# Scores of a chunk in one go on two row blocks of TensorE, the output gate loaded first, and the first values read one step earlier

## The chip, the cores and the metric

The kernel runs on one core of one Trainium2 chip. The metric is the device time of one execution in microseconds (us). Before the change it is 455.31 us as the median of three runs (453.54 to 456.17). The profiled execution took 455.49 us, of which the profile's span covers 453.8 us; the engines' names are PE (TensorE; PEld is its weight load), DVE (VectorE), ACT (ScalarE), POOL (GpSimd) and SP (SyncE, which only issues transfers here).

## The reference

An xLSTM-style attention with matrix memory, followed by a mixer (token mixing, then channel mixing). All numbers are float32; there are 4 batches, 8 heads, 768 tokens and a head size of 40, so the model width is 320.

```python
for t in range(S):                       # per batch and head
    m_new  = max(f_gate[t] + m, i_gate[t])
    f_stab = exp(f_gate[t] + m - m_new);  i_stab = exp(i_gate[t] - m_new);  m = m_new
    C = f_stab * C + i_stab * outer(v[t], k[t])          # 40 x 40
    n = f_stab * n + i_stab * k[t]
    y[t] = sigmoid(o_gate[t]) * (C @ q[t]) / max(|n . q[t]|, 1)
x  = y as (B, S, 320)
h  = relu(x^T @ w_tok1) @ w_tok2          # tokens: 768 -> 256 -> 768
u  = x + h^T
out = u + relu(u @ w_ch1) @ w_ch2         # channels: 320 -> 1536 -> 320
```

## The kernel before

**Chunks and steps.** The recurrence is computed in 6 chunks of 128 tokens (`NC`, `L`). Inside a chunk the tokens attend to each other: scores = keys times queries for each head, multiplied elementwise by decays `gb` (an exponential of gate sums), then multiplied by the values. Across chunks a state `st` per head is carried. A chunk is worked in three steps, one for each group of heads: 3, 3 and 2 heads (`HEADS`), so a batch has 18 steps (`STEPS`). Step m belongs to chunk m // 3 and group m % 3.

**Scores before.** `step_scores` makes one float32 matmul per step. The stationary operand is `kd`: the keys of the group's heads stacked on 120 (or 80) rows. The moving operand is `qz`: the queries laid out as blocks on the diagonal, each head's 40 rows beside zeros, 384 (or 256) columns wide. So one matmul gives the scores of three heads, and two thirds of its products are with zeros. In the trace a float32 matmul is two PE instructions, each with its own weight load. The result goes to PSUM bank `pS`; in batch 0 steps alternate between `pS` and `pC[0]`. `scores` on DVE reads the bank and multiplies it into `gb` (L856), one instruction per step. The zeros of `qz` are written once by DVE (L784), and SP waits for that (`mem_ready`) before it loads the first keys and queries, with one transfer for `kd` and three for `qz` per chunk.

**Other work of a step on PE.** `step_state` (L1089) makes the chunk's contribution to the state in bank `pN`, for step m - 1. `step_values` makes, for step m - 2, the product of queries and state (L1113) and of scores and values: in batch 0 one float32 matmul per head (L1124), in the later batches six bf16 ones per head (L1134), for which scores and values are split into three bf16 pieces by ACT (L628, L604), POOL (L494, L496) and DVE (`p_low`, L865).

**What runs beside what.** Every engine has a fixed list of instructions and works it in order; semaphores tie them. Batch 0's attention runs alone, up to about 51.6 us: there `spread_decays` (L1042, L1046) puts the decays into PSUM by matmul and ACT takes exponentials (L676), three steps ahead (`LEAD`). The attention of batch b + 1 is then spread over the mixer of batch b: for b = 0 all of it over the mixer's 24 slots, and for b = 1, 2 step 0 lies ahead of the second token matmul, step 1 inside it, and the others in slots 0 to 15. A slot is one tile of the hidden channel layer: `hidden` (8 matmuls, L1236 to L1241), then one attention step, then `project` of the slot before (9 matmuls, L1165); ACT and DVE split the hidden tile into two pieces between them (L760, L988). So 18 chunks of attention lie in mixers, and 6 stand alone.

**The start.** ACT issues the load of batch 0's output gate `o_gate` (two parts) and its first large instruction is the sigmoid of it (L580), ahead of all exponentials in ACT's list. DVE and POOL compute running sums of the gates on 32 rows in three segments (L794 maxima, L802 sums, L469 to L486 on POOL). PE runs idle matmuls (`keep_warm`, L1015) while it waits: 19, 5 and 10 of them at three places.

Of the kernel before, what the change touches and what calls it, by code (L numbers as in the profile page):

```python
# [50 lines left out]
FIRST_VALUES_AT = 6  # L51
# [8 lines left out]
WARM_START, WARM_NEXT, WARM_THIRD = 19, 5, 10  # L60
# [21 lines left out]
def program(nc, qT, kT, kvN, i_gate, f_gate, o_gate, w_tok1, w_tok2, w_ch1, w_ch2, out):  # L82
    ctx = ExitStack()
    with ctx:
# [25 lines left out]
        kd = sb("kd", [ROWS, R, NG, L])  # L110
        qz = sb("qz", [ROWS, R, NG, GH, L])
# [53 lines left out]
        def scores_bank(ba, m):  # L165

            return [pS, pC[0]][m % 2] if ba == 0 else pS
# [21 lines left out]
        mem_ready = sem("mem_ready")  # L189
# [114 lines left out]
        QK_DMAS = 4  # L304
# [4 lines left out]
        def _(sp):  # L309
# [3 lines left out]
            def load_scores(ba, c):  # L313

                n = NC * ba + c
                r = c % R
                if n >= R:
                    sp.wait_ge(s_mm, NG * (n - R + 1))
                ready = qk_in[r]
                queries = qT[ba, c]  # L320
                sp.dma_start(kd[:, r], kT[ba, c]).then_inc(ready, 16)
                for j in range(GH):
                    rows_j = slice(j * D, (j + 1) * D)
                    sp.dma_start(qz[rows_j, r, :, j, :], queries[rows_j, :, :]).then_inc(ready, 16)
# [60 lines left out]

            load_values(0, 0)
            sp.wait_ge(mem_ready, 1)
            load_scores(0, 0)
# [385 lines left out]
        def _(dve):  # L774
# [9 lines left out]
            nc.vector.memset(qz[:, :, :, :, :], 0.0).then_inc(mem_ready, 1)  # L784
# [63 lines left out]
            def scores(ba, m):  # L848

                c, g = divmod(m, NG)  # L850
                k = STEPS * ba + m
                n = HEADS[g]
                tile = gb[:, c % Q, GH * g:GH * g + n, :]
                dve.wait_ge(s_mm, k + 1)
                dve.wait_ge(e_exp, k + 1)
                nc.vector.tensor_tensor(tile, scores_bank(ba, m)[:, 0:n * L].rearrange("p (h t) -> p h t", h=n), tile,  # L856
                                        ALU.mult).then_inc(p_ready, 1)
# [10 lines left out]
            def state(ba, m):  # L868
# [6 lines left out]
                sums = pN[0:n * D, 0:n * E1].rearrange("p (h e) -> p h e", e=E1)  # L875
# [49 lines left out]
            def attention(ba, m):  # L925
# [3 lines left out]
                if 1 <= m <= STEPS - NG:  # L929
                    state(ba, m - 1)  # L930
# [77 lines left out]
        def _(pe):  # L1008
# [58 lines left out]
            def step_scores(ba, m):  # L1067

                c, g = divmod(m, NG)
                k = STEPS * ba + m  # L1070
                n, r = HEADS[g], c % R
                if g == 0:
                    pe.wait_ge(qk_in[r], 16 * QK_DMAS * (ba * (NC // R) + c // R + 1))
# [3 lines left out]
                mm(scores_bank(ba, m)[:, 0:n * L], kd[0:n * D, r, g, :],  # L1077
                   qz[0:n * D, r, g, 0:n, :].rearrange("p h t -> p (h t)"),
                   start=True, stop=True).then_inc(s_mm, 1)

            def step_state(ba, m):
# [5 lines left out]
                if ks != 0:  # L1087
                    pe.wait_ge(n_read, ks)
                mm(pN[0:n * D, 0:n * E1], kv[:, r, GH * g * D:(GH * g + n) * D],  # L1089
# [49 lines left out]
            def attention(ba, m):  # L1139

                if m < STEPS:
                    step_scores(ba, m)
# [10 lines left out]
                if 1 <= m <= STEPS - NG:  # L1153
                    step_state(ba, m - 1)
# [150 lines left out]
```

## Time and profile before

| what | value |
|---|---|
| time, median of 3 | 455.31 us (453.54 to 456.17) |
| profiled execution / its span | 455.49 us / 453.8 us |
| PE busy (weight loads) | 439.6 us, 97% (407.6 us, 90%) |
| DVE, ACT, POOL busy | 255.6, 209.1, 208.3 us |
| chain that ended last | PE 85%, DVE 5%, issue 4%, ACT 4% |
| score matmuls (L1077) | 144 PE instructions, two for each of the 72 steps |
| DVE's product with the scores (L856) | 72 instructions |

The page gives busy times as shares of the span, and the chain that ended last, traced back from the last instruction. A busy PE is not PE at its peak: a matmul's recorded duration holds its latency, and neighbours overlap. What one costs in a dense stretch is read from start to start. Two starts in a timeline give that.

### The profile page before, as it was taken

What the parts mean: (1) busy time and instruction counts of PE and PEld (TensorE: products, weight loads), DVE (VectorE), ACT (ScalarE), POOL (GpSimd) and SP (SyncE); (2) the same over time, 40 slices, a digit from 0 to 9 for tenths busy, and PEclk for the clock granted to TensorE, in tenths of its full rate; (3) what the DMA queues carried; (4) which work ended last, traced back from release to release, by engine and by line L of the source; (5) the groups of instructions that cost most, each with busy time, mean ns of one, the idle gap of its engine ahead of it and who ended that gap; (6) DMA issues with size and microseconds to landing.
All of it is one profiled execution on the core that took longest, in us unless ns stands there. A gap on an engine that the chain in (4) does not pass through costs nothing.

```text
span 453.8 us, 9518 instructions
## 1 busy us (share of the span) xinstructions
PE 439.6 (97%) x3463; PEld 407.6 (90%) x3463; DVE 255.6 (56%) x592; ACT 209.1 (46%) x517; POOL 208.3 (46%) x293
## 2 busy tenths in 40 slices
PE   8899999999999999899999999999999999999996
PEld 3588988999999989799999998899999998999996
DVE  7689865777765356776674237666665326213122
ACT  3666459666554247654552137655652213211120
POOL 7535421789886333888861204798883000000000
PEclk9899999999999999999999999999999999999999
DMA  7557990443344415434454013534310010000101
GB/s 211 195 168 217 348 263 27 119 129 111 103 131 146 127 43 166 143 92 131 124 154 143 1 44 102 150 120 142 126 61 1 1 43 2 0 1 0 46 1 43
DMA packets 36616, 47.38 MB, mean 104 GB/s; under 512 B 3356, under 2 KB 29082, under 8 KB 36570
## 3 DMA queue, kind: packets, MB, share of 16 engines
q1 hardware_dynamic: 35674, 45.76, 33.4%
q10 hardware_dynamic: 896, 1.02, 0.6%
q8 instruction: 28, 0.46, 0.5%
q14 instruction: 18, 0.15, 0.1%
HBM read 42.73 MB, written 4.03 MB: 103 GB/s over the span
## 4 chain that ended last, share of the span: by engine, by line
PE 85%; DVE 5%; issue 4%; ACT 4%; DMA 1%; DVEq 0%; POOL 0%; POOLq 0%; ACTq 0%
PE pC L1165 32%; PE pA L1236 7%; PE pA L1237 7%; PE pA L1238 7%; PE pS L1077 6%; PE pA L1165 5%; PE pY L1134 4%; PE pA L1240 3%; PE pA L1241 3%; PE pC L1015 2%; PE pY L1113 2%; PE pN L1089 2%; DVE gb L856 1%; PE pA L1195 1%; DMA x<-o_gate_dram 1%
## 5 line engine op out<-in xcount | busy, mean ns | idle before, releaser
L988 DVE SCALAR_TENSOR_TENSOR h_lo<-pA,h_hi 128x384 fp32r<-128x384 f32 x96 | 53.5, 557 | 147.9 <-ACT h_hi L760 147.9
L760 ACT ACTIVATE h_hi<-pA 128x384 fp32r<-128x384 f32 x96 | 46.8, 488 | 138.7 <-PE pA L1241 138.6
L1165 PE MATMUL pC<-wc_hi,h_hi 128*128 128x320 f32 x288 | 94.1, 327 | 1.1 <-DVE wc_lo L846 1.0
L1165 PE MATMUL pC<-wc_lo,h_hi 128*128 128x320 f32 x288 | 88.7, 308 | 0.0
L1165 PE MATMUL pC<-wc_hi,h_lo 128*128 128x320 f32 x288 | 88.4, 307 | 0.0
L494 POOL TENSOR_TENSOR gb<-gb,pb 128x384 f32<-128x384 f32 (+1 forms) x54 | 49.1, 909 | 63.9 <-ACT pb L628 63.4
L1236 PE MATMUL pA<-uT_hi,wc_hi 128*128 128x384 f32 x192 | 65.2, 340 | 0.3 <-DVE wc_lo L846 0.3
L1237 PE MATMUL pA<-uT_lo,wc_hi 128*128 128x384 f32 x192 | 64.7, 337 | 0.0
L1238 PE MATMUL pA<-uT_hi,wc_lo 128*128 128x384 f32 x192 | 64.3, 335 | 0.0
L1165 PEld LDWEIGHTS pC<-wc_hi,h_hi 128*128 128x128 f32 x288 | 54.0, 188 | 2.3 <-DVE h_lo L988 1.3
L1165 PEld LDWEIGHTS pC<-wc_lo,h_hi 128*128 128x128 f32 x288 | 54.2, 188 | 0.1
L1165 PEld LDWEIGHTS pC<-wc_hi,h_lo 128*128 128x128 f32 x288 | 54.0, 188 | 0.0
L618 ACT ACTIVATE gb<-gb,aT 128x128 f32<-128x128 f32 x144 | 47.4, 390 | 1.5 <-POOL gb L504 1.5
L1077 PE MATMUL pS<-qz,kd 120*128 120x384 f32 (+1 forms) x126 | 47.2, 455 | 0.5 <-DVE gb L856 0.5
L628 ACT ACTIVATE pb<-gb 128x384 bf16<-128x384 f32 (+1 forms) x54 | 26.3, 487 | 34.2 <-DVE gb L856 33.8
L865 DVE TENSOR_TENSOR pb<-gb,pb 128x384 bf16<-128x384 f32 (+1 forms) x54 | 38.1, 706 | 0.6
L526 POOL TENSOR_TENSOR x_lo<-x,x_hi 128x320 fp32r<-128x320 f32 x24 | 21.5, 897 | 33.3 <-ACT x_hi L652 33.3
L1236 PEld LDWEIGHTS pA<-uT_hi,wc_hi 128*128 128x128 f32 x192 | 36.2, 188 | 0.5 <-issue 0.5
L1238 PEld LDWEIGHTS pA<-uT_hi,wc_lo 128*128 128x128 f32 x192 | 36.1, 188 | 0.0
L1237 PEld LDWEIGHTS pA<-uT_lo,wc_hi 128*128 128x128 f32 x192 | 36.0, 188 | 0.0
L496 POOL CAST pb<-gb 128x384 bf16<-128x384 f32 (+1 forms) x54 | 31.4, 582 | 3.5
L856 DVE TENSOR_TENSOR gb<-pS,gb 128x384 f32<-128x384 f32 (+1 forms) x63 | 31.7, 503 | 1.2 <-PE pS L1077 0.8
(135 smaller groups left out, 881.6 us busy)
## 6 DMA issues: line engine op xcount, KB each, us to landing
gb<-g_dram SPq DMA_DIRECT2D x18, 512.0 KB, 3.9
kv<-kvN_dram SPq DMA_DIRECT2D x24, 324.0 KB, 4.0
kd<-kT_dram SPq DMA_DIRECT2D x24, 180.0 KB
qz<-qT_dram SPq DMA_DIRECT2D x72, 60.0 KB
out_dram<-u SPq DMA_DIRECT2D x24, 160.0 KB, 1.9
qd<-qT_dram SPq DMA_DIRECT2D x20, 180.0 KB, 2.6
gq<-g_dram SPq DMA_DIRECT2D x45, 60.0 KB
wc_raw<-w_ch_dram SPq DMA_DIRECT2D x6, 384.0 KB, 6.1
```

The costliest lines, as they stand in the source:

```text
L494: nc.gpsimd.tensor_tensor(tile, tile, pb[:, g, 0, 0:HEADS[g], :], ALU.subtract).then_inc(p_rest, 1)
L496: nc.gpsimd.tensor_copy(pb[:, g, 1, 0:HEADS[g], :], tile).then_inc(p_mid, 1)
L618: last = nc.scalar.activation(tile, tile, ACT.Exp, bias=aT[:, c, bass.ds(head, 1)])
L760: nc.scalar.activation(h2[0][:, slot % 2], pA[slot % 2][:, 0:HALF], ACT.Relu).then_inc(h2_hi, 1)
L856: nc.vector.tensor_tensor(tile, scores_bank(ba, m)[:, 0:n * L].rearrange("p (h t) -> p h t", h=n), tile, ALU.mult).then_inc(p_ready, 1)
L865: nc.vector.tensor_tensor(pb[:, g, 2, 0:n, :], gb[:, c % Q, GH * g:GH * g + n, :], pb[:, g, 1, 0:n, :], ALU.subtract).then_inc(p_split, 1)
L988: nc.vector.scalar_tensor_tensor(h2[1][:, slot % 2], pA[slot % 2][:, 0:HALF], 0.0, h2[0][:, slot % 2].bitcast(F32), ALU.max, ALU.subtract) ...
L1077: mm(scores_bank(ba, m)[:, 0:n * L], kd[0:n * D, r, g, :], qz[0:n * D, r, g, 0:n, :].rearrange("p h t -> p (h t)"), start=True, stop=True) ...
L1165: ins = mm(dst, a[p], b[q], start=first and n == 0, stop=last and n == 2)
L1236: mm(dst, wc1[0][:, t, f], uh[:, t, cols], start=t == 0, stop=False)
L1237: mm(dst, wc1[0][:, t, f], ul[:, t, cols], start=False, stop=False)
L1238: mm(dst, wc1[1][:, t, f], uh[:, t, cols], start=False, stop=False)
```

## The change

- Keys and queries are sent by the host in one array `kq_pairs`, with even heads on partitions 0 to 39 and odd heads on partitions 64 to 103 of a new tile `kq`; `kd`, `qz` and the memset of zeros are gone, and a chunk's load is 2 transfers of 40 partitions in place of 4.
- `chunk_scores` replaces `step_scores`: at the first step of a chunk it makes 8 float32 matmuls, one per head, each with 40 rows, 128 stationary and 128 moving columns, alternately on the upper and lower 64 rows. Even heads go to bank `pS`, odd heads to `pC[0]` in batch 0 and to `pN`, the state's bank, later. One semaphore count for all 8.
- It waits until DVE has read all scores of the chunk before; from batch 1 on also until DVE has read that chunk's states from `pN`.
- DVE reads each step's scores with two instructions, one for each bank.
- From batch 1 on the state matmuls move: none in a chunk's first step, group 0's in the second, groups 1 and 2 in the third (`states_in`, `state_place`), with waits both ways between scores and states in `pN`.
- SP waits for both parts of `o_gate` before it loads chunk 0's scores and values, in this order.
- `WARM_THIRD` goes from 10 to 8, and `FIRST_VALUES_AT`, the step at which DVE reads chunk 0's values, from 6 to 5.

```diff
-FIRST_VALUES_AT = 6
+FIRST_VALUES_AT = 5
-WARM_START, WARM_NEXT, WARM_THIRD = 19, 5, 10
+WARM_START, WARM_NEXT, WARM_THIRD = 19, 5, 8
...
-        kd = sb("kd", [ROWS, R, NG, L])
-        qz = sb("qz", [ROWS, R, NG, GH, L])
+        kq = sb("kq", [128, R, 2, H // 2, L])
...
+        def scores_place(ba, head):
+            pair, odd = divmod(head, 2)
+            return (pC[0] if ba == 0 else pN) if odd else pS, pair * L
+        def state_place(ba, g):
+            col = L if ba > 0 and g == NG - 1 else 0
+            return pN[0:HEADS[g] * D, col:col + HEADS[g] * E1]
+        def states_in(ba, m):
+            if ba == 0:
+                return [m - 1] if 1 <= m <= STEPS - NG else []
+            c, g = divmod(m, NG)
+            if c >= NC - 1 or g == 0:
+                return []
+            return [m - 1] if g == 1 else [m - 1, m]
...
-                    sp.wait_ge(s_mm, NG * (n - R + 1))
+                    sp.wait_ge(s_mm, n - R + 1)
-                sp.dma_start(kd[:, r], kT[ba, c]).then_inc(ready, 16)
-                for j in range(GH):
-                    sp.dma_start(qz[rows_j, r, :, j, :], queries[rows_j, :, :]).then_inc(ready, 16)
+                for odd in range(2):
+                    sp.dma_start(kq[64 * odd:64 * odd + D, r], kq_pairs[ba, c, odd]).then_inc(ready, 16)
...
+            sp.wait_ge(o_in[0], 16)
+            load_scores(0, 0)
+            sp.wait_ge(o_in[1], 16)
             load_values(0, 0)
-            sp.wait_ge(mem_ready, 1)
-            load_scores(0, 0)
...
-            nc.vector.memset(qz[:, :, :, :, :], 0.0).then_inc(mem_ready, 1)
...                                                   # DVE, scores(ba, m)
-                dve.wait_ge(s_mm, k + 1)
+                dve.wait_ge(s_mm, NC * ba + c + 1)
+                if ba > 0 and c < NC - 1 and g > 0:
+                    dve.wait_ge(n_mm, NG * (NC - 1) * ba + NG * c + (1 if g == 1 else NG))
                 dve.wait_ge(e_exp, k + 1)
-                nc.vector.tensor_tensor(tile, scores_bank(ba, m)[:, 0:n * L]..., tile, ALU.mult).then_inc(p_ready, 1)
+                for odd in range(2):
+                    heads = [h for h in range(GH * g, GH * g + n) if h % 2 == odd]
+                    ...
+                    last = nc.vector.tensor_tensor(tile, sums, tile, ALU.mult)
+                last.then_inc(p_ready, 1)
...                                                   # PE
-            def step_scores(ba, m):
-                held = 2 if ba == 0 else 1
-                if k >= held:
-                    pe.wait_ge(p_ready, k - held + 1)
-                mm(scores_bank(ba, m)[:, 0:n * L], kd[0:n * D, r, g, :],
-                   qz[0:n * D, r, g, 0:n, :]..., start=True, stop=True).then_inc(s_mm, 1)
+            def chunk_scores(ba, c):
+                n = NC * ba + c
+                if n > 0:
+                    pe.wait_ge(p_ready, NG * n)
+                if ba > 0:
+                    pe.wait_ge(n_read, states(ba, c - 1))
+                for head in range(H):
+                    pair, odd = divmod(head, 2)
+                    rows = slice(64 * odd, 64 * odd + D)
+                    last = mm(scores_of(ba, head), kq[rows, r, 0, pair, :], kq[rows, r, 1, pair, :],
+                              start=True, stop=True)
+                last.then_inc(s_mm, 1)
...                                                   # PE, step_state(ba, m)
+                if ba > 0:
+                    pe.wait_ge(p_ready, STEPS * ba + NG * c + (1 if g == 0 else 2))
+                    if g > 0:
+                        pe.wait_ge(n_read, NG * (NC - 1) * ba + NG * c + 1)
...                                                   # PE, attention(ba, m)
-                if m < STEPS:
-                    step_scores(ba, m)
+                if m < STEPS and m % NG == 0:
+                    chunk_scores(ba, m // NG)
```

PE's list in a mixer slot that holds the first step of a chunk (batch 1), before. `pS` and `pN` are the score and state banks, `pY` the values' bank.

```order
L1241 MATMUL pA<-uT_hi,wc_lo 128x384
L1077 MATMUL pS<-qz,kd 128x384
L1089 MATMUL pN<-vw,kv 80x82
L1113 MATMUL pY<-st,qd 128x123
L1134 MATMUL pY<-vb,pb 128x41 x18
```

The same place after the change.

```order
L1273 MATMUL pA<-uT_hi,wc_lo 128x384
L1104 MATMUL pS<-kq 128x128
L1104 MATMUL pN<-kq 128x128
L1104 MATMUL pS<-kq 128x128
L1104 MATMUL pN<-kq 128x128
L1104 MATMUL pS<-kq 128x128
L1104 MATMUL pN<-kq 128x128
L1104 MATMUL pS<-kq 128x128
L1104 MATMUL pN<-kq 128x128
L1145 MATMUL pY<-st,qd 128x123
L1166 MATMUL pY<-vb,pb 128x41 x18
```

One matmul of 384 columns became eight of 128, the two later steps of the chunk have none, and the state matmul left this slot for the chunk's third step.

DVE's list in batch 0 from the third step of chunk 2 to the first of chunk 3, before (`gb` holds the decays and takes the product, `stn` and `st` are the state).

```order
L856 TENSOR_TENSOR gb<-pS,gb 128x256
L886 TENSOR_TENSOR stn<-pN,blocks 120x123
L895 SCALAR_TENSOR_TENSOR st<-st,gq,stn 120x123
L846 TENSOR_TENSOR wt_lo<-wt_raw,wt_hi 128x768
L856 TENSOR_TENSOR gb<-pC,gb 128x384
```

The same stretch after.

```order
L880 TENSOR_TENSOR gb<-pS,gb 128x128
L880 TENSOR_TENSOR gb<-pC,gb 128x128
L910 TENSOR_TENSOR stn<-pN,blocks 120x123
L919 SCALAR_TENSOR_TENSOR st<-st,gq,stn 120x123
L863 TENSOR_TENSOR wt_lo<-wt_raw,wt_hi 128x768
L880 TENSOR_TENSOR gb<-pS,gb 128x2x128
L880 TENSOR_TENSOR gb<-pC,gb 128x128
```

Each product with the scores is two instructions; their elements are as many as before, and what stands between them is unchanged.

SP's list at the start, before.

```order
L311 DMA u<-i_gate_dram 32x640
L346 DMA kv<-kvN_dram 128x648
L321 DMA kd<-kT_dram 120x384
L324 DMA qz<-qT_dram 40x3x128 x3
L321 DMA kd<-kT_dram 120x384
L324 DMA qz<-qT_dram 40x3x128 x3
L346 DMA kv<-kvN_dram 128x648
```

And after; the first `kq` transfer waits for the gate's first part, the first `kv` for its second.

```order
L330 DMA u<-i_gate_dram 32x640
L340 DMA kq<-kq_pairs_dram 40x1024 x2
L362 DMA kv<-kvN_dram 128x648
L340 DMA kq<-kq_pairs_dram 40x1024 x2
L362 DMA kv<-kvN_dram 128x648
```

The first values and scores are issued behind the output gate's landing, and eight key and query transfers became four.

## Rows read from the trace of the kernel before

**Rows 1.** The page, first part: busy us, share of the span, instructions.

```profile
PE 439.6 (97%) x3463; PEld 407.6 (90%) x3463; DVE 255.6 (56%) x592; ACT 209.1 (46%) x517; POOL 208.3 (46%) x293
```

**Rows 2.** Busy time by stage: stretch and its length, each engine, PE's clock, DMA.

```profile
0.00:19.73 19.73, 16.14 (x71) 7.12 (x71) 13.49 (x23) 8.87 (x22) 12.45 (x30) 0.91 0.74 220
19.73:51.57 31.84, 31.42 (x250) 26.25 (x251) 28.13 (x74) 19.62 (x56) 15.20 (x16) 1.00 0.68 215
201.03:213.61 12.58, 12.58 (x119) 11.92 (x117) 7.86 (x21) 6.89 (x18) 10.40 (x15) 1.00 0.41 127
```

**Rows 3.** Timeline of PE in mixer slots: start, duration, engine, instruction, count, idle before.

```profile
98.70 0.81 PE L1077 MATMUL pS<-qz,kd 120*128 120x384 f32 x2
99.35 0.31 PE L1089 MATMUL pN<-vw,kv 128*80 128x82 f32 x2
...
107.14 0.60 PE L1077 MATMUL pS<-qz,kd 80*128 80x256 f32 x2
107.57 0.37 PE L1089 MATMUL pN<-vw,kv 128*120 128x123 f32 x2
```

**Rows 4.** Timeline of PE's weight loads in batch 0's attention.

```profile
34.44 0.75 PEld L1124 LDWEIGHTS pY<-kv,gb 128*128 128x128 f32 x6
35.11 0.30 PEld L1077 LDWEIGHTS pS<-qz,kd 120*128 120x128 f32 x2
```

**Rows 5.** Timeline of PE: matmuls on 32 rows beside ones on 128.

```profile
23.92 0.22 PE L1029 MATMUL pC<-ident,pb 32*128 32x32 f32 x1
23.98 0.22 PE L1030 MATMUL pC<-ident,u 32*128 32x32 f32 x1
24.14 0.34 PE L1042 MATMUL pA<-above,eye 128*128 128x384 bf16 x1
```

**Rows 6.** Timeline of PE at the start.

```profile
12.93 0.39 PE L1042 MATMUL pA<-above,eye 128*128 128x256 bf16 x1 [1.86 <-ACT gb L676]
...
13.33 3.69 PE L1015 MATMUL pC<-ident 128*128 128x512 bf16 x10
...
17.03 0.86 PE L1077 MATMUL pC<-qz,kd 120*128 120x384 f32 x2
...
18.86 0.42 PE L1089 MATMUL pN<-vw,kv 128*120 128x123 f32 x2
```

**Rows 7.** Timeline of ACT at the start.

```profile
8.55 1.81 ACT L580 ACTIVATE x<-x 128x1920 f32<-128x1920 f32 x1 [4.28 <-DMA x<-o_gate_dram]
...
11.99 2.21 ACT L676 ACTIVATE gb<-pA,aT 128x128 f32<-128x128 f32 x8
```

**Rows 8.** Timeline of DVE at the start.

```profile
14.01 1.00 DVE L794 TENSOR_TENSOR_SCAN u<-u 32x384 f32<-32x384 f32 x1
17.93 0.56 DVE L856 TENSOR_TENSOR gb<-pC,gb 128x384 f32<-128x384 f32 x1 [2.93 <-PE pC L1077]
19.32 0.28 DVE L882 TENSOR_TENSOR st<-pN,blocks 120x123 f32<-120x123 f32 x1 [0.83 <-PE pN L1089]
19.53 0.94 DVE L802 TENSOR_TENSOR_SCAN pb<-carry,u 32x384 f32<-32x384 f32 x1
```

**Rows 9.** Timeline of POOL at the start.

```profile
16.14 0.98 POOL L473 TENSOR_TENSOR u<-u 32x384 f32<-32x384 f32 x1
```

**Rows 10.** Timeline of DVE in batch 0's attention.

```profile
33.21 0.42 DVE L856 TENSOR_TENSOR gb<-pS,gb 128x256 f32<-128x256 f32 x1
33.55 0.28 DVE L886 TENSOR_TENSOR stn<-pN,blocks 120x123 f32<-120x123 f32 x1
...
35.09 0.55 DVE L856 TENSOR_TENSOR gb<-pC,gb 128x384 f32<-128x384 f32 x1
35.55 0.23 DVE L886 TENSOR_TENSOR stn<-pN,blocks 80x82 f32<-80x82 f32 x1
```

**Rows 11.** Timeline of DVE, last piece of a step's scores.

```profile
211.73 0.57 DVE L865 TENSOR_TENSOR pb<-gb,pb 128x384 bf16<-128x384 f32 x1
```

**Rows 12.** Timeline of PE: values matmuls that need such pieces.

```profile
188.47 0.62 PE L1134 MATMUL pY<-vb,pb 128*128 128x41 bf16 x18 [0.78 <-DVE pb L865]
...
208.60 0.81 PE L1077 MATMUL pS<-qz,kd 120*128 120x384 f32 x2
...
213.61 0.56 PE L1134 MATMUL pY<-vb,pb 128*128 128x41 bf16 x16
```

More of the change, by code:

```diff
@@ L79, in step_in, with program @@
     return slot - BEHIND if b == 0 else slot + AHEAD
-def program(nc, qT, kT, kvN, i_gate, f_gate, o_gate, w_tok1, w_tok2, w_ch1, w_ch2, out):
+def program(nc, kq_pairs, qT, kvN, i_gate, f_gate, o_gate, w_tok1, w_tok2, w_ch1, w_ch2, out):
     ctx = ExitStack()
@@ L163, in program, with scores_of @@
         pN = bank("pN")
-        def scores_bank(ba, m):
-            return [pS, pC[0]][m % 2] if ba == 0 else pS
+        def scores_place(ba, head):
[4 more added lines that the diff above has]
+            return pN[0:HEADS[g] * D, col:col + HEADS[g] * E1]
+        def scores_of(ba, head):
+            where, col = scores_place(ba, head)
+            return where[:, col:col + L]
         def turned_bank(s):
@@ L303, in program @@
         O_PARTS = ((0, NC - 2), (NC - 2, NC))
-        QK_DMAS = 4
+        QK_DMAS = 2
         GQ_DMAS = 3
@@ L852, in scores @@
                 n = HEADS[g]
-                tile = gb[:, c % Q, GH * g:GH * g + n, :]
-                dve.wait_ge(s_mm, k + 1)
+                dve.wait_ge(s_mm, NC * ba + c + 1)
+                if ba > 0 and c < NC - 1 and g > 0:
+                    dve.wait_ge(n_mm, NG * (NC - 1) * ba + NG * c + (1 if g == 1 else NG))
                 dve.wait_ge(e_exp, k + 1)
-                nc.vector.tensor_tensor(tile, scores_bank(ba, m)[:, 0:n * L].rearrange("p (h t) -> p h t", h=n), tile,
-                                        ALU.mult).then_inc(p_ready, 1)
+                for odd in range(2):
+                    heads = [h for h in range(GH * g, GH * g + n) if h % 2 == odd]
+                    tile = gb[:, c % Q, heads[0]:heads[-1] + 1:2, :]
+                    where, col = scores_place(ba, heads[0])
+                    sums = where[:, col:col + len(heads) * L].rearrange("p (h t) -> p h t", t=L)
+                    last = nc.vector.tensor_tensor(tile, sums, tile, ALU.mult)
+                last.then_inc(p_ready, 1)
             def p_low(ba, m):
@@ L928, in attention @@
                     scores(ba, m)
-                if 1 <= m <= STEPS - NG:
-                    state(ba, m - 1)
+                for done in states_in(ba, m):
+                    state(ba, done)
                 c = chunk_at(ba, m, 0) if (ba, m) != (0, NG - 1 + FIRST_LAG) else None
@@ L1086, in step_state @@
                 pe.wait_ge(v_weighed, (NC - 1) * ba + c + 1)
-                if ks != 0:
+                if ba == 0 and ks != 0:
                     pe.wait_ge(n_read, ks)
-                mm(pN[0:n * D, 0:n * E1], kv[:, r, GH * g * D:(GH * g + n) * D],
+                if ba > 0:
+                    pe.wait_ge(p_ready, STEPS * ba + NG * c + (1 if g == 0 else 2))
+                    if g > 0:
+                        pe.wait_ge(n_read, NG * (NC - 1) * ba + NG * c + 1)
+                mm(state_place(ba, g), kv[:, r, GH * g * D:(GH * g + n) * D],
                    vw[:, c % 2, GH * g:GH * g + n, :].rearrange("p h e -> p (h e)"),
@@ L1152, in attention @@
                                 spread_query_decays(k // NG + 1)
-                if 1 <= m <= STEPS - NG:
-                    step_state(ba, m - 1)
+                for done in states_in(ba, m):
+                    step_state(ba, done)
                 if lag(ba) <= m < STEPS + lag(ba):
@@ L1289 @@
     arrays = {
-        "qT": rows(q), "kT": rows(k),
+        "kq_pairs": np.ascontiguousarray(np.stack([paired(k), paired(q)], axis=4)),
+        "qT": rows(q),
         "kvN": np.ascontiguousarray(np.concatenate([tokens(k).reshape(B, S, DM), values.reshape(B, S, H * E1)], axis=2)),
```

16 lines of the change are left out of this document (5 added, 11 removed).

## The prediction

> **What bounds the kernel now.** I read the busy times first [rows 1]: PE is busy 97% of the span, no other engine over 56%. The stages [rows 2] say where that holds. In a mixer with attention laid over it (201.03 to 213.61, one chunk of three slots) PE is busy for all 12.58 us at full clock, POOL 10.40, DVE 7.86, so a microsecond less of PE's list there is a microsecond of the end, until POOL or a chain through it takes over. In batch 0's attention (19.73 to 51.57) PE is busy 31.42 of 31.84 us but DVE 28.13, and DVE's dependent instructions leave gaps of their own, so two engines bound it and relief for one alone is worth little. In the first 19.73 us PE works 16.14 us, of which most are idle matmuls: that stage is bound by waits, read below.
>
> **The overlapped chunks: PE.** A chunk's scores cost PE, from start to start, 0.65 us for each group of three heads (98.70 to 99.35) and 0.43 for the group of two (107.14 to 107.57) [rows 3]: 1.73 us a chunk. That is the columns: 2 x 384 + 256 = 1024, at 1.69 ns each. After the change the columns are 8 x 128 = 1024 again. Were all eight matmuls to follow one another, nothing would be saved; everything hangs on whether those on the lower and upper 64 rows run side by side, which no row of this trace shows.
>
> Bounds. A float32 matmul is two instructions, and where its moving side is narrow the trace shows the pace of its loads of 128 columns: six from 34.44 to 35.11, 0.112 us each [rows 4]. 128 moving columns take 0.108 us per instruction (0.43/256 x 128 / 2), hidden behind the next load. So 16 instructions in single file are 1.79 us, and 8 on each half side by side 0.90. A change of the row block size costs something as well: after the matmuls on 32 rows the next wide one starts 0.16 us later where the spacing among them is 0.06 [rows 5], 0.10 more. I take 0.09 on the way in and again out, 0.18 a chunk. Scores then cost 1.08 us a chunk side by side (saves 0.65) and 1.97 in single file (loses 0.24). The far end below is the column time halved without any switch, 0.87. The far end above is loads that are not hidden inside a block either, 16 x (0.112 + 0.108) + 0.18 = 3.70, which loses 1.97 a chunk; all rows on 128 rows show loads hidden, so I give that end no more than a trace of chance.
>
> I take side by side. The nearest rows are matmuls on one block only, so the trace does not choose; the reason is the layout: the halves use disjoint rows of the array and of the memory, and write different banks. 18 chunks x 0.65 = 11.7 us.
>
> The Trainium skill speaks on both sides here. "TensorEngine Tiling (Array Packing)", Tiling Modes, says that tiles operate independently, and that weight loads and matmuls of different tiles can run in parallel; by it the sum is the 1.08 us a chunk above. It also says there that changing the tiling mode drains the engine; by that rule, the trace agrees, with the 0.10 us. "TensorE: Matmul & The Clock Gate", LDWEIGHTS, says that a load's time goes by its columns and not by its rows. The trace's 0.112 us agrees, and it speaks against this change: 16 loads of 128 columns replace 6, and if loads are served one at a time the sum is the single file, 1.97 us.
>
> **What is given back there.** Scores must still pass ACT, POOL and DVE before PE multiplies them with values two slots on. For a chunk's first group PE now reaches that point sooner: from 208.60 to 213.61 [rows 12] lie 5.0 us with two score matmuls in them (0.65 + 0.43), which go, and one more state matmul comes in (82 columns at 1.69 ns, 0.14), so 4.1 us remain. The piece that ends last is done at 211.73 + 0.57 = 212.30 [rows 11], 1.3 us ahead of 213.61, so 0.4 us is left in a settled chunk: no wait. Early in a batch there is no room: at 188.47 PE already waited 0.78 us for it. There the 0.9 us comes back as wait, in 3 batches 2.7 us, and I add 0.8 for batch 1's other early chunks, whose room is under 1 us: 3.5 us given back. Bounds: 0 if DVE and POOL move up with PE, and 18 x 0.4 = 7 if every chunk falls short by half.
> POOL's 10.40 us in 12.58 [rows 2] still fits into 11.93. DVE's extra instructions (below) are 0.2 us against 4.7 us of room. The states' move costs nothing where I can see: the same number, in a slot that lost a 0.43 us matmul. The new waits of the scores (last chunk's products and states read) hold back the 8 matmuls and all of PE's list behind them; DVE does those in the slot before, and a whole `project` and `hidden` of PE lie between.
>
> **The start.** ACT's sigmoid begins at 8.55 after 4.28 us of waiting for the output gate, and the first exponentials follow at 11.99 [rows 7]; PE waits 1.86 us for them until 12.93, its clock falls (0.91 granted in this stage [rows 2]) and the 10 idle matmuls take 3.7 us at 1.2 GHz before its list goes on to 17.03 and 18.86 [rows 6]. DVE meanwhile stands idle 2.93 and 0.83 us for PE's scores and state [rows 8]. With the gate's transfers alone on the queues its landing moves up; the bounds are 0 and the 4.28 us, and I take 2, since about half of what moved in that time was queued beside it. Then the exponentials end near 11, PE loses its wait, its clock stays up, and 8 idle matmuls end before 14. DVE's next long step, the sum at 19.53, is then held by POOL's L473, which ends at 16.14 + 0.98 = 17.12 [rows 9] and itself waits for DVE's L794 at 14.01 [rows 8], which does not move. So the gain is 19.5 - 17.3 = 2.2 us, whatever more the gate gains; with no gain of the gate, two idle matmuls less give 0.85. Chunk 0's keys, queries and values are issued only once the gate is there, near 6.5; they cost nothing while the scores are done before 12, because PE waits for the exponentials until then anyway.
>
> **Batch 0's attention.** DVE's product takes 0.46 us from start to start for 384 elements and 0.34 for 256 [rows 10], so a further instruction costs 0.07 to 0.10. One more in each of 16 steps behind the start: 1.1 to 1.6 us, I take 1.3. It is not hidden, since DVE binds. PE's saving is. The alternation of two banks is gone: PE makes a chunk's scores only once DVE has read the last ones, 1.1 us plus signals, and DVE has one state (0.6 us) and mostly a weight split or chunk 0's values, now at step 5, to do meanwhile, over 1.5 us together. Cost 0 side by side; in single file 2.0 us are not covered, 0.6 us in each of three chunks, 1.9.
>
> **The sum** against the profiled 455.5 us: -11.7 + 3.5 - 2.2 + 1.3 = -9.1, so 446.4. The profiled execution stands 0.2 us above the median, nothing beside the rest. Transfers (DMA share 0.41 in a chunk [rows 2]) and the removed memset of zeros, which ran before DVE had input, cost and bring nothing.
>
> **The rivals.**
> 1. *Single file.* The two blocks' loads are served one after another. For it: the pace of 0.112 us in rows 4 is the load's, not the matmul's, and each pair of instructions on one block comes together, so the blocks alternate only every second one. Against it: the disjoint rows. Price: 18 x 0.24 = 4.3 us, batch 0 1.9 + 1.3, start -2.2: 455.5 + 5.3 = 460.8, slower. It decides from a cost of about 1.7 us a chunk upward.
> 2. *Half side by side.* Only where the block changes does a load or matmul hide: 12 of 16 places, 1.34 + 0.18 = 1.52 us a chunk, saves 0.2 x 18 = 3.8, gives back 1, and -0.9 from the start and batch 0: 451.8.
> 3. *The chains take it.* Side by side, but the path over ACT, POOL and DVE falls behind in every chunk (7 us given back, and another 1 in batch 0): 455.5 - 11.7 + 8 - 0.9 = 450.9. For it: POOL would be busy 10.40 of 11.93 us, and waits for ACT in between.
> 4. *The start brings nothing*, because the landing of the gate does not move: 446.4 + 1.4 = 447.8, inside the forecast's own range.
>
> **How the numbers follow.** Forecast 0.50 (with rival 4), own range 443 to 449; rival 1 0.22, rival 2 0.14, rival 3 0.12, others 0.02. The range of 8 in 10 leaves 0.05 below 442 and reaches up into rival 1: 442 to 461. A measurement of this kernel tells about 0.5%, 2.3 us: faster is under 453.0. That is 0.50 + 0.12 + 0.10 of rivals 2 and 3 and their spread, less a little: 0.69. Same is what is left of them and the mildest of rival 1: 0.08. Slower 0.23.
>
> **What would show it.** In the profile after: in a mixer slot with scores, the eight matmuls from the first start to the next instruction of other kind in 1.1 us (right), 1.5 (rival 2) or 2.0 (rival 1); starts of neighbouring instructions on different halves closer than 0.1 us. A settled chunk lasts 11.9 us instead of 12.6; if it lasts more while the scores take 1.1, the wait stands before the values matmuls, released by DVE's last piece (rival 3). ACT's sigmoid begins near 6.5; DVE's sum of the third segment at about 17.3. The forecast is wrong if scores cost over 1.3 us, or if PE's waits for pieces exceed 5 us in all.

## The result: 3.2% slower, and the profile after

The changed kernel takes 469.4 us (median of 4 runs, 469.1 to 470.39) against 455.18 (453.54 to 456.17) of the one before: a ratio of 1.032, 95% interval 1.029 to 1.035. Forecast were 446.4 us and a range of 442 to 461. In some of the experiments below single executions of one kernel differ by much (13 us in e3, 26 in e4, 15 in e7), the longer ones at a lower mean clock, and the ratios leave those out, so I give the times as well.

The page of the changed kernel, profiled at 470.39 us with a span of 468.6: busy times, and PE's granted clock in tenths over the span in 40 slices.

```profile
PE 450.7 (96%) x3701; PEld 427.3 (91%) x3701; DVE 249.8 (53%) x663; ACT 208.2 (44%) x517; POOL 208.0 (44%) x293
...
PEclk9755558999999999999999999999999999999999
```

PE is busy 11.1 us longer than in [rows 1], though it was to have less to do, and the clock's row says where: four slices of 11.7 us at half, and parts of their neighbours. The stages, each with its length, the busy time of PE, PEld, DVE, ACT and POOL, then the granted clock, DMA share and GB/s:

```profile
10.00:17.30 7.30, 6.26 (x58) 4.61 (x58) 5.74 (x13) 6.05 (x24) 4.84 (x6) 1.00 0.96 313
17.30:19.18 1.88, 0.02 (x1) 0.03 (x1) 1.85 (x5) 0.73 (x2) 0.93 (x2) 0.86 0.70 275
19.18:50.00 30.82, 30.82 (x188) 28.55 (x190) 17.02 (x55) 12.14 (x36) 8.66 (x11) 0.50 0.37 117
50.00:68.10 18.10, 18.10 (x101) 17.16 (x98) 10.34 (x32) 5.41 (x13) 5.80 (x6) 0.50 0.68 232
68.10:73.20 5.10, 5.10 (x20) 5.10 (x21) 4.31 (x8) 1.94 (x3) 1.02 (x1) 0.50 1.02 299
```

Up to 17.3 us the clock is full. Then PE stands idle, and from the next instruction on, for 54 us, it works without a pause at 0.50, the lower of its two levels (1.2 GHz); before, the same attention ran at 1.00 [rows 2]. Batch 0's token matmuls start at 68.10 instead of 51.40, and the clock comes back only among them, at 73 us. What PE waited for is read from PE's timeline, then DVE's (start, duration, engine, instruction, count, idle before it and its releaser):

```profile
16.56 0.76 PE L1156 MATMUL pY<-kv,gb 128*128 128x41 f32 x6
19.18 0.55 PE L1104 MATMUL pS<-kq 40*128 40x128 f32 x1 [1.86 <-DVE gb L880]
```
```profile
16.78 1.73 DVE L819 TENSOR_TENSOR_SCAN pb<-carry,u 32x384 f32<-32x384 f32 x1 [1.00 <-POOL u L491]
18.54 0.29 DVE L880 TENSOR_TENSOR gb<-pS,gb 128x128 f32<-128x128 f32 x1
18.75 0.28 DVE L880 TENSOR_TENSOR gb<-pC,gb 128x128 f32<-128x128 f32 x1
```
```profile
16.71 0.99 POOL L492 TENSOR_TENSOR u<-u 32x384 f32<-32x384 f32 x1
```

Chunk 1's scores, all eight heads, may start only when DVE has multiplied the last of chunk 0's. In DVE's list these two products stand behind the sum of the third segment, which itself waits 1.00 us for POOL and takes 1.73. Before, it took 0.94 [rows 8]; now POOL's L492 runs beside it. In the ten traces in which POOL works beside this sum it takes 1.73 or 1.74 us, in the four in which POOL is idle (before, e6, e9, e12) 0.93 or 0.94. By that an estimate of what this overlap costs is 0.8 of PE's 1.86 us. The kernel before had its scores in two banks in turn and never waited there. This is the start of the trouble; that it is the cause took the experiments.

The start did move: sigmoid at 7.39, exponentials at 10.83, the sum at 16.78 instead of 8.55, 11.99 [rows 7] and 19.53 [rows 8]. The sum's end moved less than its start: 18.51 instead of 20.47.

```profile
7.39 1.80 ACT L598 ACTIVATE x<-x 128x1920 f32<-128x1920 f32 x1 [2.87 <-DMA x<-o_gate_dram]
...
10.83 2.17 ACT L694 ACTIVATE gb<-pA,aT 128x128 f32<-128x128 f32 x8
```

And the two blocks do work side by side. A settled chunk's scores in a mixer, PE's timeline:

```profile
221.61 0.34 PE L1272 MATMUL pA<-uT_hi,wc_hi 128*128 128x384 f32 x1
221.78 0.34 PE L1273 MATMUL pA<-uT_hi,wc_lo 128*128 128x384 f32 x1
222.05 0.37 PE L1104 MATMUL pS<-kq 40*128 40x128 f32 x1
222.06 0.37 PE L1104 MATMUL pN<-kq 40*128 40x128 f32 x1
222.27 0.27 PE L1104 MATMUL pS<-kq 40*128 40x128 f32 x1
222.27 0.27 PE L1104 MATMUL pN<-kq 40*128 40x128 f32 x1
...
222.94 0.27 PE L1104 MATMUL pS<-kq 40*128 40x128 f32 x1
222.94 0.27 PE L1104 MATMUL pN<-kq 40*128 40x128 f32 x1
223.15 0.48 PE L1145 MATMUL pY<-st,qd 120*128 120x123 f32 x2
223.47 0.21 PE L1166 MATMUL pY<-vb,pb 128*128 128x41 bf16 x2
```

A pair starts within 0.01 us, pairs 0.11 apart: 1.09 us from the first start (222.05) to the next instruction of another kind (223.15), 1.08 forecast. But the price of changing the block size stands partly outside these bounds. The wide matmul before takes 0.27 us to the first score where its neighbour takes 0.17; the first pair takes 0.21 where the others take 0.11; the next block starts 0.20 behind the last pair; and the two state matmuls after it need 0.32 us where two such took 0.22 in the kernel before. That is 0.1 us four times, 0.39 in all, so 1.29 us for a chunk's scores, just inside the 1.3 beyond which the prediction called itself wrong. The settled chunk as a whole, same columns as the stages:

```profile
218.68:230.88 12.20, 12.20 (x129) 11.81 (x127) 7.47 (x24) 6.77 (x19) 10.40 (x16) 1.00 0.43 130
```

12.20 us against 12.58 [rows 2]; forecast 11.93. Last, PE's waits from 73 us on (releaser, us in all, times, longest):

```profile
PE pY L1166 <- DVE pb L889: 2.6, 6, 0.8
...
PE pS L1104 <- DVE st L906: 0.7, 2, 0.3
PE pY L1145 <- DVE den L935: 0.7, 1, 0.7
```

With the others 8.7 us; the same view of before sums to 5.8, of which the pieces have 1.6. So the waits for pieces rose by 1 us, and waits of new kinds (scores and state matmuls for DVE's reading of the states, the product of queries and state for its denominators) came in with 2.1; the other kinds changed little.

**Where the time went.** PE's `hidden` matmuls, which every mixer has, compare the kernels: the first one starts at 84.75 us instead of 65.71, 19.0 later, the last at 461.60 instead of 446.71, 14.9 later. So the change loses 19.0 us in batch 0 and the token matmuls behind it, and gains 4.2 from there on.

### The profile page after: what moved, and what is told of

The parts are those of the page before. It is cut to its first block, busy times and chain, and to the rows that moved or that the text cites. A ratio compares the mean times of both kernels' runs of the same rounds, so it can differ in the third digit from the quotient of the medians.

```text
span 468.6 us, 10017 instructions
## 1 busy us (share of the span) xinstructions
PE 450.7 (96%) x3701; PEld 427.3 (91%) x3701; DVE 249.8 (53%) x663; ACT 208.2 (44%) x517; POOL 208.0 (44%) x293
## 3 DMA queue, kind: packets, MB, share of 16 engines
q10 hardware_dynamic: 896, 1.02, 0.7%
## 4 chain that ended last, share of the span: by engine, by line
PE 79%; DVE 7%; ACT 6%; issue 5%; DMA 2%; POOL 0%; ACTq 0%; DVEq 0%
PE pC L1197 28%; PE pA L1269 6%; PE pA L1268 6%; PE pA L1270 6%; PE pS L1104 5%; PE pA L1197 5%; PE pY L1166 4%; PE pA L1273 3%; PE pA L1272 3%; PE pY L1145 3%; PE pN L1121 2%; PE pC L1156 2%; DVE gb L880 2%; DMA x<-o_gate_dram 2%; PE pY L1156 2%
## 5 line engine op out<-in xcount | busy, mean ns | idle before, releaser
L512 POOL TENSOR_TENSOR gb<-gb,pb 128x384 f32<-128x384 f32 (+1 forms) x54 | 45.3, 839 | 65.4 <-ACT pb L646 65.4
L514 POOL CAST pb<-gb 128x384 bf16<-128x384 f32 (+1 forms) x54 | 35.0, 648 | 3.5
L1104 PE MATMUL pS<-kq 40*128 40x128 f32 x192 | 32.2, 316 | 3.4 <-DVE gb L880 1.9
L1104 PEld LDWEIGHTS pS<-kq 40*128 40x128 f32 x192 | 27.2, 216 | 8.5 <-issue 7.5
L889 DVE TENSOR_TENSOR pb<-gb,pb 128x384 bf16<-128x384 f32 (+1 forms) x54 | 33.5, 620 | 0.6
```

What stands on the lines that cost most here:

```text
L512: nc.gpsimd.tensor_tensor(tile, tile, pb[:, g, 0, 0:HEADS[g], :], ALU.subtract).then_inc(p_rest, 1)
L514: nc.gpsimd.tensor_copy(pb[:, g, 1, 0:HEADS[g], :], tile).then_inc(p_mid, 1)
L889: nc.vector.tensor_tensor(pb[:, g, 2, 0:n, :], gb[:, c % Q, GH * g:GH * g + n, :], pb[:, g, 1, 0:n, :], ALU.subtract).then_inc(p_split, 1)
L1104: last = mm(scores_of(ba, head), kq[rows, r, 0, pair, :], kq[rows, r, 1, pair, :], start=True, stop=True)
```

## The experiments

Theory A: PE's new wait drops its clock, and batch 0's narrow matmuls do not raise it. Theory B: the scores on two blocks are too light for a full clock, wait or not. Theory C: the loss is in later chains. Theory D: the start's part alone brings it.

**e1: fill the wait.** Idle matmuls where PE stood 1.86 us.

```diff
+                            if k == 5:
+                                pe.wait_ge(gq_exp, 1)
+                                keep_warm(9)
                             if k % NG == 2 and k // NG + 1 < NC:
```

> The changed kernel, with nine idle matmuls of PE put into the place where it stood 1.86 us for DVE's product ahead of chunk 1's scores. Theory A (that stall drops PE's clock and batch 0's narrow matmuls do not raise it again): the clock stays full from 19 us on, batch 1's token matmuls start near 52 us instead of 68, and the run takes 449 us (469 less some 20; between 447 and 453). Theory B (the eight-on-two-blocks scores are themselves too light for the clock): it falls all the same, some us later, and the run takes 467 to 471. Theory C (the loss lies in the later batches' chains, the low clock in batch 0 costs little since DVE binds there): full clock in batch 0, but the run stays above 460.

Measured: 461.61 us (460.92 to 461.83), ratio 1.016 (1.013 to 1.018). The stages of e1:

```profile
19.91:31.20 11.29, 11.00 (x118) 10.04 (x118) 9.21 (x32) 7.38 (x24) 5.10 (x6) 1.00 0.39 125
31.20:32.22 1.02, 0.01 (x1) 0.04 (x1) 1.02 (x4) 0.82 (x2) 0.00 (x0) 1.00 1.05 357
32.22:34.60 2.38, 2.38 (x29) 2.19 (x29) 2.25 (x5) 0.67 (x3) 1.84 (x2) 0.94 0.79 244
34.60:59.69 25.09, 25.09 (x140) 23.84 (x141) 15.44 (x49) 8.62 (x22) 7.87 (x9) 0.50 0.64 219
```

Between A and B, and no number of theirs: the clock holds over two chunks of the new scores, which speaks against B, and falls behind the next wait of the same kind (1.02 us at 32.22, for DVE's product again). My theory A had counted one wait; there is one ahead of several chunks' scores.

**e2: take the wait away.** DVE's sum of the third segment behind the products.

```diff
+                if (ba, m) == (0, 2):
+                    gate_sums(2)
...
-                if m == 1:
-                    gate_sums(2)
```

> The changed kernel, with DVE's sum of the third segment moved behind its products of chunk 0's third group: the sum no longer stands ahead of the products that PE waits for before chunk 1's scores. Theory A (the stall drops the clock): PE's wait of 1.86 us goes or falls below 0.5 us, the clock stays full, 449 us (447 to 453). If a new stall at the state or the values behind it takes its place, the clock falls there and the run is as long as the changed kernel, 466 to 471. Theory B (scores on two blocks are too light for the clock): 467 to 471 with the stall gone. Theory C (later chains): above 460 at full clock.

Measured: 466.85 us (464.53 to 467.69), 1.027 (1.024 to 1.030). This is the second case of the expectation. The wait is gone, others take its place: 0.53 us at 20.80 for POOL, 0.21 and 0.56 at 22.87 and 23.80 for DVE, and PE is busy 3.69 of the 5 us before the fall.

```profile
20.00:25.00 5.00, 3.69 (x35) 3.13 (x34) 4.55 (x13) 3.70 (x12) 2.40 (x3) 1.00 0.28 83
...
26.00:63.80 37.80, 37.80 (x217) 35.44 (x216) 21.80 (x70) 13.51 (x36) 11.02 (x12) 0.50 0.56 191
```

So no single wait is to blame: three short ones do the same.

**e3: idle matmuls after the fall.** As e1, at `k == 8` with `pe.wait_ge(gq_exp, 2)` and `keep_warm(8)`.

> The changed kernel, with eight idle matmuls (about 3 us at the low clock) three slots later, when the clock has already fallen. The stall stays as it is. Theory A in its narrow form (batch 0's matmuls leave the clock where it is, and only a dense stretch raises it): the clock comes back behind the idle matmuls, near 27 us, and the run takes 450 to 457. If batch 0's matmuls cannot hold a full clock at all (Theory B), it comes back for a few us and falls again: 468 to 473.

Measured: ten executions from 453.55 to 466.8 us, median 462.7, three of them under 455. In the profiled one (465.5) the eight idle matmuls bring the clock back, and it falls once more at 38 us, behind a wait of 0.96:

```profile
21.00:27.00 6.00, 6.00 (x33) 4.70 (x32) 2.82 (x10) 3.70 (x12) 1.69 (x3) 0.50 0.11 25
27.00:36.00 9.00, 8.11 (x76) 6.77 (x74) 6.36 (x23) 4.72 (x13) 1.69 (x2) 0.95 0.50 165
...
39.00:66.00 27.00, 27.00 (x147) 25.75 (x146) 16.37 (x53) 8.97 (x23) 7.57 (x10) 0.50 0.67 220
```

The idle matmuls of 512 columns raise it, as A says. That the same program ends at 453.6 or 466.8 shows batch 0 on an edge: whether a wait of about 1 us drops the clock is not settled by the wait alone.

**e4: the start's part alone** on the kernel before.

```diff
-FIRST_VALUES_AT = 6
+FIRST_VALUES_AT = 5
-WARM_START, WARM_NEXT, WARM_THIRD = 19, 5, 10
+WARM_START, WARM_NEXT, WARM_THIRD = 19, 5, 8
...
-            load_values(0, 0)
+            sp.wait_ge(o_in[0], 16)
             sp.wait_ge(mem_ready, 1)
             load_scores(0, 0)
+            sp.wait_ge(o_in[1], 16)
+            load_values(0, 0)
```

> The kernel before, with the start's part of the change alone: output gate's load first, two idle matmuls fewer, chunk 0's values read a step sooner; scores as before, a group of heads at a time. Prediction's step: 2.2 us less, 453.1 us. By the trace of the changed kernel the gate came 1.2 us sooner and DVE's sum 2.8 us sooner: 452.5 to 454. If this start by itself makes PE wait at 17 to 19 us and drops the clock as in the changed kernel (theory D: the start is guilty, not the scores): 465 to 472.

Measured: ratio 0.997 (0.995 to 0.999), nine executions from 451.67 to 455.48, so about 1.2 us gained (0.3 to 2.1) where the prediction had 2.2; and one, the profiled one, at 477.51. There PE waits 0.79 us for DVE's state and the clock goes, with the old scores:

```profile
19.42 0.34 PE L1091 MATMUL pN<-vw,kv 128*80 128x82 f32 x2 [0.79 <-DVE st L884]
```
```profile
22.00:72.69 50.69, 50.69 (x211) 41.74 (x210) 26.65 (x68) 15.43 (x43) 12.14 (x13) 0.50 0.53 166
```

B falls with this: the wide scores do not keep the clock up either. D falls as the rule (nine of ten), but with the sooner start alone the clock can fall. Whether the other nine had this wait is not known; one execution was profiled.

**e7: a wait put into the kernel before**, scores and start untouched.

```diff
+                if (ba, m) == (0, 3):
+                    pe.wait_ge(gp_rest, 1)
```

> The kernel before, with PE made to wait near 21 us for a sum of POOL's that it does not need yet, about 1.9 us. Scores as before, and the start as before. Theory A (a stall drops the clock, and batch 0's matmuls leave it low, whatever their shape): 0.50 of full clock from about 22 us to the dense token matmuls; 470 to 478. Theory B (the old, wider scores would raise the clock again, the new ones cannot): back to full clock within some us, 456 to 459.

Measured: 472.8 us (467.68 to 482.55), 1.035 (1.027 to 1.043). One wait of 1.77 us costs ten times its length.

```profile
19.00:20.76 1.76, 0.00 (x1) 0.00 (x1) 1.67 (x4) 0.70 (x2) 1.38 (x2) 1.00 0.39 126
...
24.00:67.27 43.27, 43.27 (x220) 35.21 (x220) 25.68 (x67) 15.39 (x44) 10.38 (x12) 0.62 0.46 139
```

A holds, with a correction: the 0.62 is a mean. The clock fell near 22.7 us and came back near 57, still in batch 0 (0.50 from 54 to 56 us, 1.00 from 57 on). Under batch 0's matmuls it can rise; here that took some 34 us.

**e5: idle matmuls ahead of every chunk's scores.** Nine before chunk 1, five before chunks 2 to 5.

```diff
+                            if k > 2 and k % NG == 2:
+                                pe.wait_ge(gq_exp, k // NG)
+                                keep_warm(9 if k == 5 else 5)
```

> The changed kernel with idle matmuls ahead of the scores of every chunk of batch 0: nine before chunk 1, five (0.9 us at full clock) before each of chunks 2 to 5. One filled place moved the fall of the clock from 19 to 34 us, where PE waited 1.02 us for DVE's product. Theory A (each wait of about a microsecond in batch 0 drops the clock, and PE's narrow matmuls there do not raise it): no wait above 0.5 us stays before 57 us, the clock is full throughout, batch 1's token matmuls start near 50.5 us; from there on the changed kernel gains the 4.2 us that it gained from the same point of the first mixer on; 450 us (448 to 452). Theory B (the scores on two blocks are too light for the clock, wait or not): the clock falls again near 35 us, 460 to 463.

Measured: 453.05 us (450.08 to 457.22), 0.994 (0.991 to 0.997): A's number missed by 1 us, B's by 7. Two short falls were left:

```profile
22.25:25.70 3.45, 3.45 (x18) 2.48 (x17) 2.19 (x7) 2.48 (x9) 0.41 (x1) 0.51 0.09 17
25.70:50.00 24.30, 23.77 (x234) 20.50 (x232) 21.30 (x69) 13.13 (x35) 8.09 (x9) 1.00 0.69 213
...
53.00:56.20 3.20, 3.20 (x14) 3.20 (x14) 2.41 (x7) 1.19 (x3) 1.48 (x2) 0.50 1.03 410
```

The first fall came behind a wait of 0.50 us for DVE's product and ended within the five idle matmuls; the second came behind 1.11 us ahead of the last chunk's values. The first is telling: up to there PE's list is that of e1, and in e1 a wait of 0.50 us at the same place (until 19.91 us, here until 19.44) left the clock up.

**e11: the same, with those two places filled.** Twelve for nine, and six more ahead of the last values.

```diff
-                                keep_warm(9 if k == 5 else 5)
+                                keep_warm(12 if k == 5 else 5)
...
+                if (ba, m) == (0, STEPS - 1):
+                    keep_warm(6)
```

> The changed kernel with idle matmuls in batch 0: twelve (not nine) before chunk 1's scores, five before each of chunks 2 to 5, and six ahead of the last chunk's values, where PE waited 1.1 us for DVE. With nine and five the clock was low from 22.3 to 25.7 us and from 53 to 56 us, behind waits of 0.5 and 1.1 us, which cost about 2 and 1.5 us. Theory A: without these two waits the clock is full throughout and the run takes 449.5 us (448 to 451). If the clock is low in the same places, another cause than the waits drops it: 452 to 454.

Measured: 451.42 us (451.1 to 458.69), 0.992 (0.989 to 0.994), 1.9 above the expectation. The clock is full, all of it by work that computes nothing:

```profile
20.00:52.00 32.00, 31.88 (x312) 27.41 (x311) 27.82 (x86) 17.78 (x49) 13.56 (x15) 1.00 0.63 201
```

The only difference between this kernel and the changed one is 38 idle matmuls more, with the waits that place them: 18 us. The first `hidden` matmul starts 0.4 us later than before, against 19.0 for the changed kernel, so the low clock, with the waits that brought it, cost 18.7 us there.

**e6 and e12: the scores' part alone.** In e6 the start's part is simply undone in the changed kernel.

> The changed kernel with the start put back as it was (output gate's load behind the values, ten idle matmuls, chunk 0's values at the old step): the scores' part alone. Theory A: PE is relieved by 0.4 us a chunk and DVE has one instruction more a step, so PE has to wait for DVE before each chunk's scores; the clock falls somewhere in batch 0, 460 to 471. Theory D (only the start's part brings the stall that drops the clock, the scores alone do not): full clock, 451 to 453.

Measured: 471.95 us (470.3 to 472.41), 1.036 (1.030 to 1.042), but not a clean test. The sigmoid came late:

```profile
13.04 1.80 ACT L596 ACTIVATE x<-x 128x1920 f32<-128x1920 f32 x1 [8.78 <-DMA x<-o_gate_dram]
```

The memset of zeros had held chunk 0's keys and queries back on SP's queue; without it they go ahead of the gate, whose sigmoid starts 4.5 us later than before, and PE waits 6 us. e12 puts that wait back, and the sigmoid starts at 8.86:

```diff
             load_values(0, 0)
+            sp.wait_ge(mem_ready, 1)
             load_scores(0, 0)
...
+            nc.vector.memset(kq[:, :, :, :, :], 0.0).then_inc(mem_ready, 1)
```

> The scores' part of the change alone, a second time. In the first attempt chunk 0's keys and queries were issued ahead of the output gate's load, because the memset that they waited for is gone with the scores' change; the gate landed 4.5 us later and PE waited 6 us at 17 us. Here SP waits for a memset of the keys' and queries' buffer as before (its zeros are overwritten), so the start is that of the kernel before. Theory A: the scores alone leave PE waiting for DVE in batch 0, the clock falls there, 460 to 471. Theory D (the change's start is what starts it; with the old start the clock holds in batch 0): 452 us (450 to 454).

Measured: 465.96 us (464.81 to 467.38), 1.024 (1.020 to 1.028). The waits now come later (0.39 us at 25.62, 1.26 at 32.27 for DVE's states, 1.04 at 34.60 for its product), and so does the fall:

```profile
20.00:32.00 12.00, 10.63 (x117) 9.65 (x116) 9.36 (x29) 7.61 (x26) 5.46 (x6) 1.00 0.37 111
32.00:34.60 2.60, 1.29 (x10) 1.23 (x11) 2.35 (x10) 2.00 (x5) 0.78 (x1) 0.86 0.90 294
34.60:63.50 28.90, 28.90 (x166) 27.25 (x166) 17.89 (x53) 9.27 (x24) 8.43 (x10) 0.50 0.56 194
```

The scores' part in batch 0 suffices by itself.

**e8: the lower block's four heads first, then the upper's.**

```diff
-                for head in range(H):
+                for head in [*range(0, H, 2), *range(1, H, 2)]:
```

> The changed kernel with the order of the eight heads changed: the four on the lower 64 rows first, then the four on the upper. Same instructions. If PE overlaps only neighbours in its queue, the scores of a chunk take the single file, 16 x 0.112 = 1.8 us and 0.4 for the two changes of block size, 2.2 us, against 1.3 in turn; behind batch 0 the kernel then loses 0.5 us a chunk against before. If it overlaps across the whole list, 1.3 us as in turn. In batch 0 PE has 0.9 us more work a chunk; by theory A the clock falls all the same as long as the wait at 19 us stands: 475 to 485 in all.

Measured: 483.17 us (2 runs), 1.062 (1.054 to 1.069). In between: of each block's eight instructions only three run beside the other's.

```profile
230.62 0.82 PE L1104 MATMUL pS<-kq 40*128 40x128 f32 x5
231.17 0.37 PE L1104 MATMUL pN<-kq 40*128 40x128 f32 x1
231.28 0.27 PE L1104 MATMUL pS<-kq 40*128 40x128 f32 x1
231.38 0.27 PE L1104 MATMUL pN<-kq 40*128 40x128 f32 x1
...
231.50 0.27 PE L1104 MATMUL pS<-kq 40*128 40x128 f32 x1
231.61 0.72 PE L1104 MATMUL pN<-kq 40*128 40x128 f32 x5
232.25 0.37 PE L1145 MATMUL pY<-st,qd 120*128 120x123 f32 x1
```

From first start to the next kind 1.63 us, against 1.09 in turn. The first of the upper block starts within 0.01 us of the fifth of the lower, ahead of three instructions that stand before it in the list. PE started none from further back; how far it looks in other lists is not shown. Behind batch 0 this kernel loses 4.0 us against before, where the one in turn gains 4.2.

**e9 and e10: the two blocks in batches 1 to 3 alone.** Batch 0 keeps its scores, two banks in turn (its buffer is laid over the new one). e9 with the old start, e10 with the start's part as well.

```diff
...
-                if m < STEPS and m % NG == 0:
+                if ba == 0 and m < STEPS:
+                    step_scores(m)
+                if ba > 0 and m < STEPS and m % NG == 0:
                     chunk_scores(ba, m // NG)
...
```

> The kernel before, with the scores of eight heads on two blocks in batches 1 to 3 alone. Batch 0 keeps its scores by groups of heads in two alternating banks, and its start. Theory A (the loss sits in batch 0, whose PE waits drop the clock; from the first mixer on the change gains): full clock, batch 1's token matmuls start near 51.4 us as before, and then the gain seen behind that point, 4.2 to 4.7 us: 450.5 us (449.5 to 452), a ratio of 0.990. Theory C (later chains take it all): 454 to 456.

> As the run before in this list (eight heads on two blocks in batches 1 to 3 alone), with the start's part of the change as well: output gate's load first, eight idle matmuls, chunk 0's values a step sooner. The start alone gave 0.3% and in one execution of ten a low clock and 477 us. So 449.5 us where the clock holds, and some executions near 472.

Measured: e9 450.94 us (450.06 to 451.6), 0.991 (0.988 to 0.994); e10 449.85 (449.17 to 450.42), 0.988 (0.985 to 0.991). Stages of e9:

```profile
17.00:50.00 33.00, 32.54 (x258) 26.67 (x256) 28.64 (x75) 20.30 (x60) 15.65 (x17) 1.00 0.66 203
```

PE is busy 32.54 of 33.00 us, and the clock stays up. Both numbers came as expected, but for the executions near 472: none in six. Both beat both kernels. Part of e9's number is luck: in the profiled executions it is 4.6 us ahead of the kernel before, and 1.3 of that stands ahead of the first token matmul (50.14 us, expected 51.4), because the clock did not fall at the start as it did before (PE's second scores start at 15.41 us instead of 17.03); behind the first `hidden` matmul it gains 3.4, not 4.2 to 4.7. They hold counterexamples too: in e9 PE waits 1.93 us at the start, as before in [rows 6], and the clock is full behind it (1.00 from 13 to 17 us); in e10 it waits 1.27 us at 25.76 for a DMA, and the clock stays full.

## Why the prediction was wrong

That the two blocks work side by side was read rightly. The sum failed on a term that was not in it, what PE's waits do to its clock in batch 0, and even without that it asked for twice the gain that came (8.2 us behind batch 0, 4.2 measured).

- **Step that failed:** "Cost 0 side by side" in batch 0, where DVE had over 1.5 us "to do meanwhile". DVE had that, but what I asked was what DVE loses, not what PE does in that time: it stands still. The prediction itself says that DVE binds batch 0 and that relief for PE is worth little there [rows 2]. It did not go on to say that a relieved PE becomes an idle PE, and it assumed the clock. The warning was among its rows: after 1.86 us of waiting PE ran most of its idle matmuls at 1.2 GHz [rows 6]. Shown by e11 (idle work for the waits: 18 us back), e7 (a wait into the old kernel: 18 us lost) and e9 (old batch 0: no loss).
- **Scores, 1.08 us a chunk:** the pace was right, the switch mis-sized. It costs 0.39 us a chunk, not 0.18, because I took the 0.10 of [rows 5] once each way and it comes twice each way. A chunk saves 0.43 us instead of 0.65: 7.7 us over 18, not 11.7. That the eight matmuls themselves took 1.09 us against 1.08 forecast is in part chance, as the forecast counted the whole switch in it and it holds only half.
- **Given back, 3.5 us:** 7.7 less the 4.2 that arrive is 3.5. So this term is a remainder and not measured by itself. PE's waits rose by 2.9, only 1 of that for pieces, which the prediction had as the whole. By the stages a settled chunk got only 0.38 us shorter (12.58 to 12.20), 6.8 over 18, and then 2.6 is given back, close to the waits.
- **Start, -2.2 us:** the landmarks came (7.39 for 6.5, 16.78 for 17.3), alone worth 1.2 us (e4), and 1.1 ahead of the old batch 0 (e9 to e10). The term was counted from the sum's start, which came 2.75 us sooner; its end came 1.96 sooner, because the sum took 0.79 longer beside POOL.
- **Batch 0, DVE:** start and batch 0 together were to bring -0.9; at a full clock they cost 0.4 (e11), and 1.9 more than the old batch 0 with the same start (first `hidden` matmul of e11 against e10, 66.08 and 64.22). How much of the 1.9 is DVE's further instructions and how much the idle matmuls was not told apart.
- **The removed memset** was put at nothing. It held a queue: with the old start its removal makes the sigmoid of the gate start 4.5 us later (e6). The change's own waits for the gate hide that.
- **The sum** with measured terms: 18.7 (clock) + 0.4 (start and batch 0) - 7.7 (scores) + 3.5 (given back) = 14.9, and the profiled executions differ by 14.9 (470.39 less 455.49). This is bookkeeping and no test: the third and fourth term are one measured number, the 4.2 us.

Rivals 1 and 2 (single file, half) are refuted by the pairs' starts; rival 3 by the settled chunk of 12.20 us with no wait in it; rival 4 by e4. None of the four was the case. Open is why one wait drops the clock and another does not: 1.93 us in e9 and 1.27 in e10 left it up, 0.79 in e4 took it down, 0.50 took it down in e5 and not in e1, and in e3 the same program goes either way.

## What to carry to other kernels

Where another engine binds a stage, making PE's part shorter turns its work into waits; where its clock falls behind them, as here, that costs far more than the saving. Put such a saving where PE binds, and leave or fill the other stage (e10 against the changed kernel: 19.6 us). Whenever a wait or a buffer in turn is taken out, ask what PE does in that time, and what the wait had held back on its queue.

## What the runs showed of the hardware

- Behind waits of 0.5 to 2.2 us in batch 0, PE's granted clock fell from 2.4 to 1.2 GHz, in the changed kernel and e8 within the wait, in e1, e3, e4, e5 and e7 1.5 to 2.9 us after PE had gone on, and stayed there up to 54 us although PE was busy all that time (19.18 to 73.2 us in the changed kernel). It came back in the dense token matmuls, within five to eight idle matmuls of 512 columns (e5, e3), and once among batch 0's own after 34 us (e7). Waits of the same length did not always drop it: 0.50 us in e1, 1.27 in e10, 1.93 in e9.
- Float32 matmuls of 40 rows on the lower and upper 64 rows ran in pairs, both in 0.112 us, if they alternate; with four of each in a row, only three instructions of each block overlapped (e8), and the first of the upper block started ahead of three of the lower that stand before it in PE's list.
- Each change between matmuls on 128 rows and on a 64-row block cost 0.2 us, half of it ahead of the first instruction on the new block size and half behind that one (four times 0.1 us at 221.8 to 223.5 us).
- DVE's running sum over 32x384 took 0.94 us alone and 1.73 while POOL worked on 32x384 beside it.
